# A mixture-of-experts kernel on one core: the second expert's weights are loaded during the last group of the stage before

## What is computed

```python
kv = einsum('bhsd,bhse->bhde', k, v); out = einsum('bhsd,bhde->bhse', q, kv)
x = out / sqrt(mean(out * out) + 1e-6) * g_norm        # laid out as [4608, 512]
h = relu(x @ w_in); x = (h * h) @ w_out                # w_in [512, 2048], w_out [2048, 512]
logits = x @ w_gate + modality_bias[modality_id]       # 8 experts
e_idx = argmax(logits); gate = softmax(logits)[e_idx]
for e in range(8):                                     # w1 [8, 512, 1024], w2 [8, 1024, 512]
    out[e_idx == e] = gate * (relu(x[e_idx == e] @ w1[e]) @ w2[e])
```

## Time and profile before

| | us |
|---|---|
| median of 3 runs | 1402.18 (1401.32 to 1407.2) |
| the profiled execution, its own time | 1402.4 |
| its span, first to last instruction | 1400.5 |
| PE busy | 1371.1 (98% of the span) |
| DVE, ACT, POOL busy | 791.9, 591.6, 498.1 |
| mean granted TensorE clock | 0.996 of full speed |

### The profile page before, as it was taken

How to read it: one execution, slowest core, us unless ns; L and a number is a source line. 1 busy time by engine, 2 the same in 40 slices (tenths; PEclk the granted TensorE clock), 3 DMA queues, 4 the chain that set the end, 5 groups by cost and what they waited for, 6 DMA issues and landing times. The chain is left out here.

```text
span 1400.5 us, 20900 instructions
## 1 busy us (share of the span) xinstructions
PE 1371.1 (98%) x7063; PEld 1112.8 (79%) x7063; DVE 791.9 (57%) x1677; ACT 591.6 (42%) x1201; POOL 498.1 (36%) x589
## 2 busy tenths in 40 slices
PE   5999999999999999999999999998999999999998
PEld 5788888888888888887888887876788878888876
DVE  3456474474574573574574655546555555555555
ACT  3443334234233243333333343334555555555553
POOL 2643232232232132132132134504555555555551
PEclk9999999999999999999999999999999999999999
DMA  9634547557556556567474464778995113851270
GB/s 236 168 106 154 184 126 195 185 122 204 172 132 198 175 126 207 171 123 222 155 147 155 149 151 148 203 264 200 349 356 193 47 47 113 301 203 47 67 263 20
DMA packets 178917, 237.45 MB, mean 170 GB/s; under 512 B 57838, under 2 KB 97166, under 8 KB 178834
## 3 DMA queue, kind: packets, MB, share of 16 engines
q1 hardware_dynamic: 164530, 214.84, 51.9%
q0 software_dynamic: 9472, 19.96, 4.4%
q10 hardware_dynamic: 4832, 1.57, 0.6%
HBM read 148.07 MB, written 89.30 MB: 169 GB/s over the span
## 5 line engine op out<-in xcount | busy, mean ns | idle before, releaser
L664 POOL TENSOR_TENSOR stage<-stage,stage_hi 128x512 f32<-128x512 f32 x128 | 169.2, 1322 | 558.8 <-ACT stage_hi L1142 558.6
L1478 DVE TENSOR_TENSOR g_sb<-g_sb 128x512 f32<-128x512 f32 x144 | 102.1, 709 | 328.0 <-ACT g_hi L1206 323.3
L1204 ACT ACTIVATE g_sb<-ps_h 128x512 f32<-128x512 f32 x144 | 85.9, 596 | 436.5 <-DVE g_lo L1482 242.2
L809 PE MATMUL ps_h<-xT_hi,weights 128*128 128x512 f32 (+1 forms) x580 | 232.1, 400 | 0.0
L809 PE MATMUL ps_y<-g_hi,weights 128*128 128x512 f32 x576 | 231.6, 402 | 0.0
L811 PE MATMUL ps_h<-xT_hi,weights 128*128 128x512 f32 (+1 forms) x580 | 225.9, 390 | 0.0
L810 PE MATMUL ps_h<-xT_lo,weights 128*128 128x512 f32 (+1 forms) x580 | 225.3, 388 | 0.0
L811 PE MATMUL ps_y<-g_hi,weights 128*128 128x512 f32 x576 | 224.9, 390 | 0.0
L810 PE MATMUL ps_y<-g_lo,weights 128*128 128x512 f32 x576 | 224.7, 390 | 0.0
L1232 ACT ACTIVATE kv_sb<-ps_h 32x256 f32<-32x256 f32 x456 | 170.7, 374 | 122.2 <-PE ps_h L994 116.9
L994 PE MATMUL ps_y<-weights,xT_hi 128*128 128x512 f32 x656 | 177.1, 392 | 0.5 <-DVE xT_lo L1659 0.5
(11 more groups left out here) (267 smaller groups left out, 1744.9 us busy)
## 6 DMA issues: line engine op xcount, KB each, us to landing
stage<-in_moe_w SPq DMA_DIRECT2D x128, 256.0 KB
w_hi<-stage_hi SPq DMA_DIRECT2D x128, 256.0 KB
w_lo<-stage SPq DMA_DIRECT2D x128, 256.0 KB
weights<-w_hi SPq DMA_DIRECT2D x32, 1024.0 KB
weights<-w_lo SPq DMA_DIRECT2D x32, 1024.0 KB
rows<-y_sb SPq DMA_DIRECT2D x36, 256.0 KB
k_sb<-in_k SPq DMA_DIRECT2D x30, 288.0 KB, 4.6
v_sb<-in_v SPq DMA_DIRECT2D x30, 288.0 KB, 5.4
```

Source lines behind the costliest of these rows:

```text
L664: pool.tensor_tensor(stage[n % 2][:, :], stage[n % 2][:, :], stage_hi[n % 2][:, :].bitcast(F32), ALU.subtract).then_inc(split_lo, 1)
L809: pe.matmul(out_ap, lhs[0], rhs[0], start=start, stop=False)
L1204: act.activation(g_sb[:, :], ps_h[c % 2][:, 0:GROUP], ACT.Relu).then_inc(h_read, 1)
L1478: dve.tensor_tensor(g_sb[:, :], g_sb[:, :], g_sb[:, :], ALU.mult).then_inc(g_done, 1)
```

## The change: what it does

`FIRST_WEIGHTS_AT` now holds pairs of expert and piece. Expert 0's pieces are loaded in other chunks than before (the first in chunk 5 in place of 8), and pieces 0 to 5 of expert 1 are loaded in chunks 9 to 15 of the same group, each over the two chunks of `w_out_sb` that `second_product` has used (`h_ps` at `2 * piece + 5`). Behind the last group SP no longer loads pieces 0 to 3 of expert 1 around the rows; after `lists_in` it loads pieces 6 and 7 alone, without a wait between them.

```diff
                     if m.c == GROUPS - 1:
-                        for piece in FIRST_WEIGHTS_AT.get(c, ()):
-                            sp.wait_ge(h_ps, m.count(CH, 2 * piece + 2))
-                            load_weights(0, 0, piece)
+                        for e, piece in FIRST_WEIGHTS_AT.get(c, ()):
+                            sp.wait_ge(h_ps, m.count(CH, 2 * piece + (2 if e == 0 else 5)))
+                            load_weights(e, e, piece)
...
-            FIRST_WEIGHTS_AT = {8: (0,), 9: (1,), 10: (2,), 11: (3,), 12: (4,), 13: (5,), 15: (6, 7)}
+            FIRST_WEIGHTS_AT = {5: [(0, 0)], 6: [(0, 1)], 7: [(0, 2)], 8: [(0, 3)], 9: [(1, 0)], 10: [(0, 4), (1, 1)], 11: [(1, 2)],
+                                12: [(0, 5), (1, 3)], 13: [(1, 4)], 14: [(0, 6)], 15: [(1, 5), (0, 7)]}
...
             sp.wait_ge(y_ps, GROUPS)
-            load_w1(1, range(2))
             for T in range(EARLY):
                 sp.wait_ge(early_row_in[T], 64)
             store_rows(Group(GROUPS - 1))
-            load_w1(1, range(2, 4))
...
             sp.wait_ge(lists_in, 16)
-            load_w2(1)
+            for piece in range(6, 8):
+                load_weights(1, 1, piece)
             sp.wait_ge(tiles_done, 1)
             for e in range(2, E):
                 load_w1(e)
```

More of the change, by code:

```diff
@@ L570, in _, with load_w1 @@
             all_groups(group)
[L572 to L577, removed]
+            def load_w1(e):
+                sp.wait_ge(h_ps, tile_before(sp, e - 1) * 2 + (GROUPS * CH + 2))
+                sp.sem_inc(passed, 1)
+                for piece in range(4):
                     at_once = 2
@@ L580, in load_w1 @@
                         sp.wait_ge(weights_in[e % 2][piece - at_once], filled(e))
-                    elif e > 1:
+                    else:
                         sp.wait_ge(weights_in[(e - 1) % 2][piece + 6], filled(e - 1))
@@ L585, in load_w2 @@
             def load_w2(e):
-                if e > 1:
-                    sp.wait_ge(y_ps, tile_before(sp, e - 1) + (GROUPS + 1))
-                    sp.sem_inc(passed, 1)
+                sp.wait_ge(y_ps, tile_before(sp, e - 1) + (GROUPS + 1))
+                sp.sem_inc(passed, 1)
                 for piece in range(4, 8):
```

## The result

| | before | changed |
|---|---|---|
| median of 12 runs, us | 1402.52 (1400.57 to 1407.20) | 1406.57 (1403.17 to 1413.27) |
| ratio to before, 95% interval | | 1.0024 (1.0015 to 1.0034) |
| profiled execution, its own time, us | 1402.4 | 1405.14 |
| mean granted TensorE clock of the profiled execution | 0.996 | 0.992 |

The change makes the kernel slower by 0.24%, within the 0.5% that I called "the same", but clear of the measurement's interval and on the other side of my forecast, and 1406.57 lies outside my range.

A forecast was written before the change was run, and what follows sets the result against it. PE's work bounds the kernel, so only its idle time could be won. Lists' wait -2.9, later tiles' waits -1.1, last group's loads 0, what follows 0: -4.0 us, from 1402.4 to 1398.4; range 1395.5 to 1403.5.

The forecast's parts named there:

- the same: Whole kernel: case of a time within about 0.5% (7 us) of the kernel before; chance 0.87.
- What bounds the kernel: Whole kernel: PE is busy 1371.1 of 1400.5 us, so moving transfers can win only its idle time.
- the ceiling of 4.64 us: From 933 us on: three PE waits sum to 4.64 us, the most this mechanism can win, 0.33%.
- The 2.9 us at the lists: Before PE's transposes of the lists: without 2 MB beside it the scatter ends sooner and the 2.9 us wait goes.
- The "read, modify, write" rival: Scatter of ids: 4-byte writes are slow by themselves, still 14 us, the lists' wait stays; 1401.8 us, chance 0.22.
- The 1.7 us: Two PE waits before later tiles' products, for DVE's low part of x: gain 1.1 us, bounds 0 and 1.7.
- DVE starts 3 us earlier: Start of the list tiles: with lists at PE by 967.1, DVE starts at 967.7, 3 us earlier.
- The loads in the last group: Weight pieces loaded earlier, from chunk 5 on, and the longer queue from 904.23: no gain, no cost to PE.
- Cost 0: Chunks from 5 on: stage loads queue up to 2.7 us behind a piece, covered by ACT's 3.66 us idle.
- I take 0 for the stall: Second tile's first product, 940.81: expert 0's piece 7 lands in time, margin 1 to 2 us, stall 0.
- the sign that the prediction named last: Head of the second tile: a new idle stretch of PE there would show the forecast wrong.
- The second rival: Second tile: expert 0's piece 7 a little late, over 2.7 us a piece, stall 0 to 4 us; 1400.5 us, chance 0.18.

The follow-up runs named there:

- e3: Kernel before, with only pieces 2 and 3 of expert 1 loaded after the lists have come, not between last rows and lists; ratio 0.9999.
- e1: Changed kernel, PE's wait for piece 7 of expert 0 moved from before the second tile's hidden part to before the first output part; ratio 0.9995.
- e8: Control: kernel before, with only PE's wait for piece 7 of expert 0 moved to before the first output part; ratio 1.0004.
- e4: Kernel before, with pieces 0 to 3 of expert 1 queued in chunk 15 behind expert 0's piece 7; ratio 0.9996.
- e5: e4 with expert 0's piece 7 queued behind the four pieces of expert 1 in chunk 15, not ahead; ratio 1.0014.
- e6: e1, with SP also waiting for tile 3's gathered rows before loading pieces 6 and 7 of expert 1; ratio 0.9994.
- e7: e4, with SP also waiting for tile 3's gathered rows before loading pieces 4 to 7 of expert 1; ratio 0.9990.
- e9: Changed kernel, expert 0's piece 7 ahead of expert 1's pieces 4 and 5, expert 1's pieces 6 and 7 held until tile 3's rows arrive; ratio 0.9992.
- e10: Repeat of e7's kernel on another chip, against the kernel before; ratio 0.9990.
- e11: Repeat of the changed kernel on another chip, against the kernel before; ratio 1.0015.
- e2: Changed kernel with chunk 15's two pieces swapped, expert 0's piece 7 ahead of expert 1's piece 5; ratio 1.0006.

## Why the prediction was wrong

**What bounds the kernel.** Right in the main. PE's idle time was all there was to win, and the ceiling of 4.64 us held: no variant's ratio is under 0.9990. The list of PE's waits left one out, 1.4 us before L1058 at 948.79, which the change couldn't take away but behind which the half clock begins.

**The 2.9 us at the lists.** Right in kind: the 2 MB held up the scatter (e3), and the wait is gone in the changed kernel. I took 10.5 us for the scatter, between 8.8 and 14.2; it was 5.9 in the changed kernel and 5.8 to 7.7 in all eleven profiles without those 2 MB. The "read, modify, write" rival, that small writes are slow by themselves, had 0.22 and is refuted for this wait; but that is no help in group 7, where the engines were full and slow beside the scatter as before.

**The 1.7 us.** "DVE starts 3 us earlier" came true in e1 (3.1 us); the step behind it didn't. The sum has no term for the rows of tile 3, which DVE turns next: it let them be there whenever the lists were. But their gather starts when the stored rows are in. I let these rows lose some of their time without the 2 MB. From SP's last issue of them to POOL's start it was 10.3 and 10.5 us with the 2 MB beside them (before, e8), and 8.7 to 10.4 in the profiles without; in e1 and the changed kernel it was 10.2 and 10.0, nearly nothing gained. And I counted no cost for pieces 6 and 7, issued together as soon as the lists are there: they run beside the gather of tile 3, which took 4.3 us to land in e1. So of the 2.9 us about 2.3 came straight back as a wait for tile 3. Even without a stall the change would have given 0.7 us (e1), not 4.0.

**The loads in the last group.** "Cost 0" for the pieces from chunk 5 on was right as far as e1 can tell. The failed step, which turned the sign, is "I take 0 for the stall": it was 2.85 us, on a margin of 1 to 2 us, and the sign that the prediction named last, an idle stretch at the head of the second tile, is what came. A piece did take about the 2.7 us that I gave it (391 GB/s from 923 to 930, 361 from 930 to 941). What was late is the start. The first piece behind the rows of group 7 was issued at 914.54 in the kernel before:

```profile
914.54 0.59 SPq L495 DMA_DIRECT2D weights<-w_lo  x1
```

In the changed kernel that was at 920.10, 5.6 us later, where I had 2.7. The issue of the rows began 2.6 us later (907.29 for 904.70), as forecast; but then it took SP 10.43 us in place of 6.77, while the engines, full all the time, ran at 147 and 234 GB/s until 917. The sum had the rows slip, not take longer. The second rival had a stall of this size, with 0.18, at 1400.5, though it laid it on the time of a piece.

**What no case had.** I priced a stall of PE at its own length, and the sum has no term for the clock. The profiles show this stall at twice its length: 2.85 us in the changed kernel went with 6.8 us more of half clock, 3.4 us of work. Stall and half clock, less the waits that went, make 1402.4 + 2.8 = 1405.2, over the 1403.5 at which my range ends. That the stall makes the half clock longer isn't shown by a run that moves one without the other: e1 takes both away.

## What to carry to other kernels

Before a transfer is put ahead of others in a queue, look up which consumer is next in that queue and by how much it is early; here piece 7 had landed some 9 us early (the engines were idle from 931, PE came at 940.8), and that slack was spent on data that was not wanted for over 40. Order by due time: with the urgent piece first, the same bytes cost nothing that could be measured (e4 against e5). And when a wait is taken away, ask what the transfers that it held back will now run beside: here the freed pieces slowed the gather of tile 3, and when they were held back, that of tile 4.

## What the runs showed of the hardware

The granted clock after a stall. Some 16 to 21 us after the last product of the first stage PE waits 1.4 us and then does 24 tiny products (L1058), some 4 us in all, in every profile but e6's. In each of these twelve a stretch at half clock starts during those products or within 1 us behind them. Without a stall at the second tile, 8 us earlier, it lasted 3.4 us (before, e1, e3, e4, e7, e8, e9, e10); with a stall of 1.9 or 2.0 us 6.8 us (e11, e2); with one of 2.9 us 10.2 us (changed). e5, with 3.1 us, had 3.4 starting within 1 us of the stall's end and then 6.8; e6, with 2.0, had 6.8 starting within 1 us of the stall's end and none at this place. Further on, PE's waits of 3.5 and 3.8 us at tile 4 (e10, e6) went with 6.8 us each and one of 1.8 at tile 3 (e4) with 3.4, but one of 2.3 at tile 3 (e1) with none. So the length of a wait alone doesn't say what it costs; what ties the two wasn't tried.

A scatter is slow beside large loads, and they beside it. From the last scatter's leaving POOL to the issue that waits for it, 4 x 128 ids took 14.2 and 13.8 us beside 2 MB of loads (before, e8) and 5.8 to 7.7 without them (eleven profiles). And in group 7, where the scatter runs beside weights and stores, full DMA engines moved between 67 and 234 GB/s; that the scatter is what slows them there is read from their coming together, as no run has these loads and stores without it. The length of that slump differs from run to run (128 GB/s from 910 to 917 in e6), and it sets when everything behind it in the queue lands. The Trainium skill, "DMA: Bandwidth & Descriptors", Back-pressure in remote DMA, says of transfers between cores that stalled writes stall the other queues of the same engine. By that rule loads and scatter would hold each other up here too; the stretches above agree, on one core, though no run separates the queue from the engine.
